# Doing the last feature pair of a fused spectral and feed-forward kernel per block of 128, with its output stored in two halves

## The reference

```python
def reference(**kwargs):
    ...
    attn_out = _attn_ref(**attn_kwargs)      # rfft over 3008, complex mix, soft threshold, irfft
    B, S, D = attn_out.shape                 # 2, 3008, 256
    x = attn_out.reshape(B * S, D)
    x = _moe_ref(x=x, **moe_kwargs)          # h = x @ w_in; g = h * cos(h); g @ w_out
    return _moe2_ref(x=x, **moe2_kwargs)     # h = x @ w_in; g = h * clip(h + 3, 0, 6) / 6; g @ w_out
```

## Time and profile before

| | us |
|---|---|
| median of 3 runs | 1226.36 |
| lowest and highest of them | 1225.87, 1226.87 |
| the profiled execution, its own time | 1224.97 |
| span of the profiled execution | 1223.2 |
| TensorE busy in it | 1201.1 (98%) |
| VectorE, ScalarE, GpSimd busy | 605.6, 630.7, 560.0 |
| mean granted TensorE clock, share of full speed | 0.996 |

### The profile page before, as it was taken

The page is one execution under the profiler, slowest core; times in us unless marked ns, Lnnn a source line. Parts: engine busy times, 40 slices in busy tenths (PEclk is TensorE's granted clock), DMA queues, the critical chain, the costliest instruction groups (busy, mean ns, idle before and its releaser), DMA issues.

```text
span 1223.2 us, 14601 instructions
## 1 busy us (share of the span) xinstructions
PE 1201.1 (98%) x5576; PEld 1010.2 (83%) x5576; DVE 605.6 (50%) x596; ACT 630.7 (52%) x703; POOL 560.0 (46%) x294
## 2 busy tenths in 40 slices
PE   8999989899999999999999999999999999999998
PEld 8888679798888888888888888888888888888886
DVE  2787727655435435445355344454354454454444
ACT  2677646665545445445545445454454544455433
POOL 2677556675444443444434444334444344443410
PEclk9999989999999999999999999999999999999999
DMA  9388533000000100100001001001001001000000
GB/s 270 118 250 226 143 113 126 18 1 1 31 1 1 35 1 0 34 0 31 3 0 34 0 0 34 0 0 34 0 0 34 0 0 34 0 11 8 1 18 18
DMA packets 26133, 49.76 MB, mean 41 GB/s; under 512 B 3139, under 2 KB 9923, under 8 KB 25963
## 3 DMA queue, kind: packets, MB, share of 16 engines
q1 hardware_dynamic: 26098, 49.29, 13.2%
HBM read 31.06 MB, written 18.32 MB: 40 GB/s over the span
## 4 chain that ended last, share of the span: by engine, by line
PE 95%; DVE 2%; DMA 1%; ACT 1%; issue 0%; POOL 0%; SPq 0%; DVEq 0%; ACTq 0%
PE banks L578 41%; PE banks L627 41%; PE banks L483 2%; PE banks L503 2%; PE banks L499 2%; PE banks L498 2%; PE banks L556 2%; PE banks L518 1%; PE banks L519 1%; DMA v<-y_spill 1%; PE banks L468 1%; DMA y_spill<-y 0%; PE banks L534 0%; PE banks L531 0%; PE banks L532 0%; DVE phase L951 0%
## 5 line engine op out<-in xcount | busy, mean ns | idle before, releaser
L1112 POOL TENSOR_TENSOR gal<-ga,gah 128x1024 fp32r<-128x1024 f32 (+1 forms) x93 | 221.6, 2383 | 515.4 <-ACT gah L792 515.4
L947 DVE SCALAR_TENSOR_TENSOR phase<-phase,banks 128x1024 f32<-128x1024 int32 (+1 forms) x96 | 114.9, 1197 | 273.6 <-ACT phase L776 273.6
L1118 POOL TENSOR_TENSOR gbl<-gb,gbh 128x1024 fp32r<-128x1024 f32 (+1 forms) x88 | 206.6, 2347 | 16.6 <-ACT gbh L826 16.6
L784 ACT ACTIVATE cosine<-phase,half_pi 128x1024 f32<-128x1024 f32 (+1 forms) x96 | 109.1, 1136 | 192.8 <-DVE phase L951 192.1
L776 ACT ACTIVATE phase<-banks 128x1024 int32<-128x1024 f32 (+1 forms) x96 | 97.0, 1011 | 155.5 <-PE banks L578 154.8
L969 DVE TENSOR_TENSOR ga<-banks,cosine 128x1024 f32<-128x1024 f32 (+1 forms) x96 | 115.4, 1202 | 104.8 <-ACT cosine L784 97.2
L1010 DVE SCALAR_TENSOR_TENSOR gb<-ramp,banks 128x1024 f32<-128x1024 f32 (+1 forms) x96 | 115.1, 1199 | 103.8 <-ACT ramp L816 103.7
L816 ACT ACTIVATE ramp<-banks,three 128x1024 f32<-128x1024 f32 (+1 forms) x96 | 105.4, 1098 | 110.9 <-PE banks L578 110.9
L826 ACT ACTIVATE gbh<-gb 128x1024 fp32r<-128x1024 f32 (+1 forms) x96 | 100.2, 1044 | 37.2 <-DVE gb L1010 32.9
L578 PE MATMUL banks<-xl,w1h 128*128 128x512 f32 (+1 forms) x384 | 116.7, 386 | 0.0
L578 PE MATMUL banks<-xh,w_lo 128*128 128x512 f32 (+1 forms) x384 | 116.7, 385 | 0.0
(11 more groups left out here) (96 smaller groups left out, 1844.3 us busy)
## 6 DMA issues: line engine op xcount, KB each, us to landing
w<-in_w_ff SPq DMA_DIRECT2D x32, 256.0 KB, 5.9
xb<-in_x SPq DMA_DIRECT2D x32, 192.0 KB, 5.1
y_spill<-y SPq DMA_DIRECT2D x24, 256.0 KB, 2.6
xf<-x_spill SPq DMA_DIRECT2D x11, 512.0 KB, 4.3
out_y<-yt SPq DMA_DIRECT2D x11, 512.0 KB, 3.4
v<-y_spill SPq DMA_DIRECT2D x7, 780.0 KB, 7.2
x_spill<-xs SPq DMA_DIRECT2D x11, 470.0 KB, 3.2
dbs<-in_db SPq DMA_DIRECT2D x24, 128.0 KB, 3.3
```

What stands on the lines that cost most here:

```text
L784: act.activation(cosine[:, :, 0:w], phase[:, :, 0:w], ACT.Sin, bias=half_pi[:, :], scale=-1.0).then_inc(a_cos, 1)
L947: dve.scalar_tensor_tensor(out=phase[:, :, 0:w], in0=phase[:, :, 0:w].bitcast(i32), scalar=-2.0 * math.pi, in1=bank[:, at:at + 2, 0:w], op ...
L1112: pool.tensor_tensor(gal[p % 2][:, :, 0:w], ga[:, :, 0:w], gah[p % 2][:, :, 0:w].bitcast(fp32), ALU.subtract).then_inc(a_gl, 1)
L1118: pool.tensor_tensor(gbl[pb % 2][:, :, 0:w], gb[:, :, 0:w], gbh[pb % 2][:, :, 0:w].bitcast(fp32), ALU.subtract).then_inc(b_gl, 1)
```

## The change

Only the last pair (pair 95 of layer B: step 104 and what follows from it) is handled differently.

- `up` raises its semaphore (`last_h`) after each of the two blocks, not after both.
- ScalarE does `ramp` as two instructions of 128x512, then `gbh` as two. VectorE does `gb` as two, then `gbl` as two. Each waits for its block alone.
- The last `down` becomes `down_last`: the same 12 matmuls in another order. First the six of block 0 for both output halves, then the three of block 1 for c = 0, then the three for c = 1. `last_sum` rises after each output half. There is a wait ahead of each matmul that reads a high part for the first time in its group or reads a low part: eight waits in all.
- `yt` is written as two instructions of 128x512, one for each output half, and stored by two DMAs of 256 KB, each issued when its half is there.
- Six semaphores more.

```diff
@@ sync, the end
-            for tile in range(TILES - 3, TILES):
+            for tile in range(TILES - 3, TILES - 1):
                 store(tile)
-            sp.wait_ge(stored, 16 * TILES)
+            for c in range(DC):
+                sp.wait_ge(yt_ready, TILES + c)
+                sp.dma_start(out[:, c, offset(TILES - 1):TOKENS], yt[:, c, :]).then_inc(stored, 16)
+            sp.wait_ge(stored, 16 * (TILES + 1))
@@ tensor
-                mm.then_inc(done, 1)
+                    if each or e == 1:
+                        mm.then_inc(done, 1)
...
+            def down_last(p, hi, lo):
+                parts = ((wh, hi), (wl, hi), (wh, lo))
+                order = [(0, n, c) for n in range(3) for c in range(DC)] + [(1, n, c) for c in range(DC) for n in range(3)]
+                for e, n, c in order:
+                    if n == 0:
+                        pe.wait_ge(last_gh, e + 1)
+                    if n == 2:
+                        pe.wait_ge(last_gl, e + 1)
+                    w, a = parts[n]
+                    at = p * PCOLS + DC * 2 * P + e * DIM + c * P
+                    mm = pe.matmul(bank[:, 6 + c, :], w[1][:, at:at + P], a[:, e, :], start=False,
+                                   stop=(e == 1 and n == 2))
+                    if e == 1 and n == 2:
+                        mm.then_inc(last_sum, 1)
@@ scalar
+                if live.b_last:
+                    act.wait_ge(b_g, gb_)
+                    for e in range(2):
+                        act.wait_ge(last_h, e + 1)
+                        act.activation(ramp[:, e, :], bank[:, h2_bank(gb_) + e, :], ACT.Relu, bias=three[:, :]).then_inc(last_ramp, 1)
...
+                if live.b_last:
+                    act.wait_ge(b_sum, gb_ - 1)
+                    for e in range(2):
+                        act.wait_ge(last_g, e + 1)
+                        act.activation(gbh[pb % 2][:, e, :], gb[:, e, :], ACT.Copy).then_inc(last_gh, 1)
@@ vector
+                if live.y_last:
+                    dve.wait_ge(stored, 16 * (TILES - 1))
+                    for c in range(DC):
+                        dve.wait_ge(last_sum, c + 1)
+                        dve.tensor_scalar(yt[:, c, :], bank[:, 6 + c, :], 1.0 / 6.0, None, ALU.mult).then_inc(yt_ready, 1)
...
+                if live.b_last:
+                    dve.wait_ge(b_gh, gb_)
+                    dve.wait_ge(b_gl, gb_)
+                    for e in range(2):
+                        dve.wait_ge(last_ramp, e + 1)
+                        dve.scalar_tensor_tensor(out=gb[:, e, :], in0=ramp[:, e, :], scalar=6.0,
+                                                 in1=bank[:, h2_bank(gb_) + e, :], op0=ALU.min, op1=ALU.mult).then_inc(last_g, 1)
...
+                if live.b_last:
+                    pb = (p - 1) % PAIRS
+                    for e in range(2):
+                        dve.wait_ge(last_gh, e + 1)
+                        dve.tensor_tensor(gbl[pb % 2][:, e, :], gb[:, e, :], gbh[pb % 2][:, e, :].bitcast(fp32),
+                                          ALU.subtract).then_inc(last_gl, 1)
```

More of the change, by code:

```diff
@@ L213, in mixer_program @@
         yt_ready, stored = sem("yt_ready"), sem("stored")
+        last_h, last_ramp, last_g = sem("last_h"), sem("last_ramp"), sem("last_g")
+        last_gh, last_gl, last_sum = sem("last_gh"), sem("last_gl"), sem("last_sum")
         def u_out(group, j):
@@ L281, in __init__ @@
                 self.b_first = G == LAG_B
+                self.b_last = G == STEPS_A + LAG_B - 1
+                self.sum_last = G == STEPS_A + LAG_B
+                self.y_last = G == STEPS_A + LAG_B + 1
                 self.gal_by_dve = G == 0 or G == LAG_B or G == STEPS_A - 1
@@ L569, in cosine_part, with up @@
                 half_idft1(g, 4 + (g + 1) % 4, 0, cos_done)
-            def up(layer, at_bank, p, hi, lo, w_tok, done):
+            def up(layer, at_bank, p, hi, lo, w_tok, done, each=False):
                 for e in range(2):
@@ L660, in pair @@
                     up(1, h2_bank(G - LAG_B), pb, *x2_hi_lo(t - 1 if p == 0 else t),
-                       step_width(G - LAG_B), b_h)
+                       step_width(G - LAG_B), last_h if live.b_last else b_h, each=live.b_last)
                 if live.b2:
@@ L665, in pair @@
                         pe.wait_ge(yt_ready, t - 1)
-                    down(1, 6, pb, gbh[pb % 2], gbl[pb % 2], b_gh, b_gl, G - LAG_B,
-                         step_width(G - LAG_B - 1), b_sum)
+                    if live.sum_last:
+                        down_last(pb, gbh[pb % 2], gbl[pb % 2])
+                    else:
+                        down(1, 6, pb, gbh[pb % 2], gbl[pb % 2], b_gh, b_gl, G - LAG_B,
+                             step_width(G - LAG_B - 1), b_sum)
             for G in range(2, PAIRS):
@@ L810, in pair @@
                     round_x2(t, live)
-                if live.b1:
+                if live.b_last:
[3 more added lines that the diff above has]
+                        act.activation(ramp[:, e, :], bank[:, h2_bank(gb_) + e, :], ACT.Relu, bias=three[:, :]).then_inc(last_ramp, 1)
+                elif live.b1:
                     act.wait_ge(b_h, gb_ + 1)
@@ L988, in pair @@
                 gb_ = G - LAG_B
-                if p == 2 and live.y and not live.y_done:
+                if live.y_last:
[3 more added lines that the diff above has]
+                        dve.tensor_scalar(yt[:, c, :], bank[:, 6 + c, :], 1.0 / 6.0, None, ALU.mult).then_inc(yt_ready, 1)
+                elif p == 2 and live.y and not live.y_done:
                     take_y(t, live.y_reuse)
@@ L1018, in pair @@
                     take_y(t, True)
-                if live.b1 and live.gbl_by_dve:
+                if live.b_last:
[4 more added lines that the diff above has]
+                                          ALU.subtract).then_inc(last_gl, 1)
+                elif live.b1 and live.gbl_by_dve:
                     pb = (p - 1) % PAIRS
```

## The result

The changed kernel takes 1223.02 us in the median of 13 runs (1222.03 to 1223.84), the kernel before 1225.48 (13 runs, 1224.34 to 1226.87; three of them, with a median of 1226.36, were known before the prediction). The ratio is 0.9978, with a 95% interval of 0.9971 to 0.9985. So the change is worth 2.5 us between the medians and 2.7 by the ratio (0.22% of 1225.5). The interval excludes a gain of nothing, but it lies on both sides of the bound of 0.2% that the prediction set. The prediction's sum had 2.7. The time outside the span is 1.77 us, as before (1223.17 - 1221.4), so the six semaphores and the longer code cost nothing there.

A forecast was written before the change was run, and what follows sets the result against it. TensorE, busy 98% of the span, bounds the kernel; the change acts only where the chain leaves it at the end. 0.81 + 0.32 + 0.50 + 1.05 = 2.68 us take the median from 1226.36 to 1223.7 us, range 1222.8 to 1225.5.

The forecast's parts named there:

- The prediction's sum: At the kernel's end: gains of 0.81 + 0.32 + 0.50 + 1.05 = 2.68 us, so 2.7.
- the way from the sum to the median: Profiled execution forecast at 1222.3; keeping its 1.39 us below the runs' median takes the median from 1226.36 to 1223.7 us.
- the likeliest case: Gain as summed, 2.2 to 3.0 us, since every step has slack and both stores are alone on the DMA engines; chance 0.65.
- What bounds the end: Behind the last up: TensorE idle 0.81 us, restart 0.32, then a serial 1.23 + 3.1 + 0.4 us behind the last matmul.
- The hole and the restart: Ahead of the last down TensorE stands still 0.81 us, then loses 0.32 restarting; per-block work removes both, 1.13 us.
- y by halves: After the last down: yt as two half-width instructions leaves a shorter one behind the last matmul, gaining 0.50 us.
- Two stores: Final store of y: the second 256 KB lands 2.0 us plus 0.05 after issue, where 512 KB took 3.1; gain 1.05.
- Waits in the last down: Six new waits among its matmuls cost nothing; bounds 0.3 and 1.9 us; rival that TensorE stumbles there, chance 0.07.
- The slack of `gbh` 0: In the last pair on ScalarE: queued behind ramp 1, gbh 0 is 0.65 us late, free given 1.2 us of slack.
- The span: Whole profiled execution: the end forecast near 1220.5 us, where it was 1223.2.
- The one that was counted as free: Rival on the last pair's split: ramp 1 holds gbh 0 0.65 us, so chains aren't independent; counted within the likeliest case.
- the rival "slower": In the last 10 us, longer code makes an engine wait for instructions, priced at 6.45 us, giving 1230.1; chance 0.04.

The follow-up runs named there:

- the chain alone: Against the kernel before, only the last pair's up to down goes per block in the new order; y stays one instruction and one store: ratio 0.9990 (0.9981 to 0.9999).

## Why the prediction was right, and where not

The mechanism came out as forecast. What failed are two steps behind the sum, and one term of it was too large:

- **Failed: the way from the sum to the median.** I kept the distance of 1.39 us between the profiled execution before and a median of three runs, and forecast 1223.7; measured was 1223.02. With 13 runs the kernel before has a median of 1225.48, 0.9 lower, and a distance of 0.51. For the changed kernel the distance is -0.15: its profiled execution took 1223.17, above its median, where 1222.3 was forecast. So one error of 0.9 us (the span, below) and one of 1.5 us (the distance) stand against each other. That 1223.02 lies inside the range, 0.7 us from 1223.7, is in part luck. The gain as a ratio is free of both: 0.9978 on the stated 1226.36 would be 1223.66.
- **Failed: the gain as clear of the bound.** I put 0.53 of the 0.65 of the likeliest case above 2.45 us, as if a gain of 2.7 could be told from one of 2.4. The medians show 2.46 (0.20%), the ratio 2.7 (0.22%), and its interval, 13 runs on either side, goes from 1.8 to 3.6 us. These runs can't say on which side of the bound the gain lies.
- **Too large: the landing.** 1.05 us were in the sum for the two stores, 0.95 is what the split of the store gave. Together with 1.08 for the chain (1.13 forecast) and 0.56 for `yt` (0.50 forecast) that makes 2.59, the tail's gain, where the sum had 2.68.

And the rest, term by term:

- **What bounds the end: right.** The hole and the restart (1.13) are gone; the chain alone gave 1.08. TensorE's own end moved by 1.12, from 6.57 to 5.45 us after the last `up` (1218.44 - 1211.87, 1218.00 - 1212.55). But `yt` started 0.12 us after it and not 0.02, and the landing of that execution was a little shorter (3.0 us).
- **y by halves: right in size.** 0.50 was forecast; 0.56 were measured in the tail and 0.63 at the end of `yt`. In the time of `yt`'s end two small errors cancel by luck. `yt` 0 starts 0.09 us after its sum instead of 0.02, with a queue instruction in between. But the halves overlap by 0.08 (1.30 for two of 0.69), so `yt` ends at 1218.83, 6.17 after the end of the last `up`; forecast was 1218.06 - 1211.87 = 6.19.
- **Two stores: right.** Landing 2.1 us, where the lone row of 256 KB had given 2.0 plus a seam of 0.05; the gain is 0.95 where 1.05 were in the sum. The Trainium skill's formula for a transfer (DMA: Bandwidth & Descriptors, "Anatomy of one DMA") makes it 2.6 us, but the page gives it for DMAs issued from GpSimd, a condition that the prediction left out. These stores are issued from SyncE, and for them the measured 2.1 decides. Its 3.2 for 512 KB is near the 3.0 and 3.1 of these runs.
- **Waits in the last down: right**, and now shown with 24 of them.
- **The slack of `gbh` 0: right.** Moving it changed nothing. A side sum there is wrong: by the prediction's own durations the four halves on ScalarE add 2 x (0.67 + 0.63) - (1.13 + 1.07) = 0.40 us, not 0.2 to 0.3. Nothing rests on it, for the slack is more than 1 us.
- **The sum: right.** 2.68 against a tail shorter by 2.59 and 2.64 in two profiles, and 2.7 by the ratio.
- **The span: wrong.** Forecast near 1220.5, measured 1221.4. I took all that stands ahead of the last `up` as fixed. It isn't: its end moves over 1.5 us between executions of the same work, and this one lost 0.17 us by 36 us and 0.6 us in three DMAs between 148 and 169 us. Why those DMAs take longer in one execution than in another stays open.
- **The rivals.** Of those that cost time none came about: the second store landed after 2.1 us, TensorE had no gap among the last twelve matmuls, and the time outside the span stayed at 1.77 us. The one that was counted as free did come about: `gbh` 0 started only behind `ramp` 1, 0.63 us after the last `up`, and it cost nothing. The price of the rival "slower" was read too high: TensorE's 6.45 us ahead of line 556 are in the kernel before the store and the load that stand above, to 157.69, and only 0.24 us of issue is left unexplained.

## What to carry to other kernels

Once the last product is over, no work is left in this kernel to hide anything behind: the eviction and the store behind it count in full, so split them so that the last piece is small, and order the last matmuls so that one output piece is summed early. Stop splitting where the issue of the DMAs takes longer than the pieces take to come (0.35 to 0.45 us for each here). For changes of a microsecond in a kernel of 1.2 ms, compare the stretch behind the last common instruction, not spans: the span here hid 0.8 of 2.6 us. Don't carry the distance of one profiled execution from a median of three over to a forecast; forecast the difference.

## What was not expected of the hardware

- Of two VectorE instructions of 0.69 us in a row, the second starts before the first one's recorded end (1218.14, against 1217.53 + 0.69 = 1218.22): 1.30 us for both.
- Where the chain shows a queue instruction (DVEq, ACTq) between an event and the instruction that waits for it, that starts 0.07 to 0.12 us after the event (`yt`, `ramp`, `gb`, `gbh`); where it shows none, 0.02. That the wait sits in this queue instruction is an inference.
- Stores land after 1.8 us (128 KB), 2.0 to 2.1 (256 KB) and 3.0 to 3.1 (512 KB), so between 256 and 512 KB it is about 1 us for 256 KB, and below that only 0.3 for 128 KB. The issue takes 0.53 us for 512 KB, 0.35 for 256 and for a first store of 128 KB, and 0.43 to 0.45 for one of 128 KB that follows another directly.
- The two loads of `v` that stand on the chain take 4.9 to 5.7 and 3.4 to 3.9 us in the thirteen profiles, and the store of `y` ahead of them 4.1 to 4.4. Together with the time that the chain takes to its first row of `mix` (34.8 to 35.9 us) they make nearly all of the difference between two executions up to the last `up`.
